# An mLSTM-and-two-MLPs kernel: every weight's low part moves to GpSimd, the weight rounding on ScalarE moves up within its step, and two tiles' attention pieces move one step later

## The reference, cut to what matters

```python
for t in range(S):
    m_new = np.maximum(f_gate[:, :, t] + m, i_gate[:, :, t])
    f_stab = np.exp(f_gate[:, :, t] + m - m_new); i_stab = np.exp(i_gate[:, :, t] - m_new)
    C = f_stab * C + i_stab * outer(v_t, k_t);  n = f_stab * n + i_stab * k_t
    y[:, :, t] = sigmoid(o_gate_t) * (C @ q_t) / max(|n @ q_t|, 1)
xn = x / rms(x) * rms_g                       # x: 1536 tokens of 320
x  = (silu(xn @ w_gate) * (xn @ w_val)) @ w_out     # 1536 hidden units
h  = x @ w_in
out = np.maximum(0.01 * h, h) @ w_out2              # 2048 hidden units
```

## Time and profile before

| | |
|---|---|
| time, three runs | 450.92, 450.02, 449.75 us; median 450.02 us |
| profiled execution: its own time, its span | 449.68 us, 447.9 us |
| mean granted clock of PE over the span | 0.996 |
| PE busy | 427.0 us, 95% of the span |
| PEld / DVE / ACT / POOL busy | 374.9 / 235.0 / 195.1 / 90.9 us |
| chain that ended last | PE 83%; ACT 5%; issue 4%; DVE 3%; POOL 3%; DMA 2% |

### The profile page before, as it was taken

The page is one execution under the profiler, slowest core; times in us unless marked ns, Lnnn a source line. Parts: engine busy times, 40 slices in busy tenths (PEclk is TensorE's granted clock), DMA queues, the critical chain, the costliest instruction groups (busy, mean ns, idle before and its releaser), DMA issues.

```text
span 447.9 us, 8151 instructions
## 1 busy us (share of the span) xinstructions
PE 427.0 (95%) x3202; PEld 374.9 (84%) x3202; DVE 235.0 (52%) x442; ACT 195.1 (44%) x428; POOL 90.9 (20%) x92
## 2 busy tenths in 40 slices
PE   2869989999999999999999999999999999999997
PEld 1758889999878878887888888998999999999996
DVE  7676666566649555555633335354334333543534
ACT  1758485455536435234333225554343343333332
POOL 1459685122111112000433102540000000000000
PEclk9989999999999999999999999999999999999999
DMA  5867581133303050000222200310000000010101
GB/s 169 299 235 236 156 304 51 75 123 122 122 1 121 1 173 1 1 0 0 66 64 69 61 0 15 118 32 0 1 0 1 0 2 0 10 50 1 59 1 59
DMA packets 10756, 31.37 MB, mean 70 GB/s; under 512 B 1328, under 2 KB 3088, under 8 KB 10720
## 3 DMA queue, kind: packets, MB, share of 16 engines
q1 hardware_dynamic: 10720, 30.87, 21.2%
HBM read 28.85 MB, written 2.02 MB: 69 GB/s over the span
## 4 chain that ended last, share of the span: by engine, by line
PE 83%; ACT 5%; issue 4%; DVE 3%; POOL 3%; DMA 2%; POOLq 0%; DVEq 0%; ACTq 0%
PE gate_ps L1033 23%; PE value_ps L1033 23%; PE out_ps L1070 9%; PE out_ps L1106 9%; PE turn_ps L1106 6%; PE out_ps L1074 3%; PE c_ps L1106 3%; PE turn_ps L1008 2%; ACT expo L486 2%; PE turn_ps L969 2%; POOL w_sb L423 1%; PE turn_ps L986 1%; ACT w_sb L539 1%; DMA expo<-decay_scratch 1%; PE c_ps L998 1%
## 5 line engine op out<-in xcount | busy, mean ns | idle before, releaser
L1033 PE MATMUL gate_ps<-x_hi,w_sb 128*128 128x512 f32 (+1 forms) x280 | 68.5, 366 | 3.8 <-DVE act_buf L811 1.9
L1033 PE MATMUL value_ps<-x_hi,w_sb 128*128 128x512 f32 (+1 forms) x280 | 68.4, 366 | 0.0
L1033 PEld LDWEIGHTS gate_ps<-x_hi,w_sb 128*128 128x128 f32 x280 | 46.9, 188 | 12.7 <-issue 3.3
L1033 PEld LDWEIGHTS value_ps<-x_hi,w_sb 128*128 128x128 f32 x280 | 47.6, 190 | 6.7 <-DVE hid L817 0.2
L559 ACT ACTIVATE h_hi<-hid 128x512 fp32r<-128x512 f32 (+1 forms) x46 | 24.6, 535 | 63.6 <-DVE hid L817 63.4
L811 DVE SCALAR_TENSOR_TENSOR act_buf<-act_buf,gate_ps 128x512 f32<-128x512 f32 (+1 forms) x46 | 26.1, 567 | 49.6 <-ACT act_buf L545 49.6
L836 DVE TENSOR_TENSOR h_lo<-hid,h_hi 128x512 fp32r<-128x512 f32 x48 | 33.2, 692 | 33.7 <-ACT h_hi L564 33.7
L1070 PE MATMUL out_ps<-h_hi,w_sb 128*128 128x512 f32 (+1 forms) x184 | 48.1, 347 | 0.0
L564 ACT ACTIVATE h_hi<-hid 128x512 fp32r<-128x512 f32 x48 | 30.3, 632 | 37.6 <-DVE hid L824 36.5
L545 ACT ACTIVATE act_buf<-gate_ps 128x512 f32<-128x512 f32 (+1 forms) x46 | 23.0, 500 | 48.6 <-PE gate_ps L1033 48.4
L1106 PE MATMUL out_ps<-w_sb,h_hi 128*128 128x320 f32 x192 | 43.0, 309 | 0.2 <-DVE h_lo L836 0.2
(11 more groups left out here) (142 smaller groups left out, 787.0 us busy)
## 6 DMA issues: line engine op xcount, KB each, us to landing
raw<-in_w SPq DMA_DIRECT2D x12, 544.0 KB, 4.4
expo<-decay_scratch SPq DMA_DIRECT2D x12, 512.0 KB, 5.3
att_sb<-in_tok SPq DMA_DIRECT2D x12, 484.0 KB, 5.0
raw<-in_w SPq DMA_DIRECT2D x16, 352.0 KB, 3.0
att_sb<-in_qk SPq DMA_DIRECT2D x24, 160.0 KB
out_y<-y_acc SPq DMA_DIRECT2D x12, 160.0 KB, 1.9
consts_sb<-in_consts SPq DMA_DIRECT2D x1, 129.5 KB, 2.5
gates_sb<-in_gates SPq DMA_DIRECT2D x1, 96.0 KB, 2.5
```

Source lines behind the costliest of these rows:

```text
L1033: last = nc.tensor.matmul(ps[:, 0:n], lhs, rhs, start=(j == 0), stop=(j == len(xs) - 1))
```

## The change

Five edits. (1) `lo_first` on DVE is gone; POOL makes block 1's low part behind the second `inverse_rms`, and `wait_lo` counts with one semaphore. (2) On POOL, `lo_weights(6)` and `inverse_rms(2)` stand ahead of `weigh_keys(3)`. (3) On ACT, `hi_weights(s + 3)` stands right behind the tangent `first1(s)` and no longer at the end of step s, and `high1(0)` stands behind `hi_weights(3)` and tile 2's first decays. (4) In `BESIDE`, tile 3's S moves from 3 to 4, tile 4's R from 8 to 9 and its O from 9 to 10 (so that its `normalise` is now `at_once`). (5) On DVE, `finish(n)` stands ahead of the second half of `scores` where both fall into one step.

```diff
@@ -32,7 +32,7 @@
 LAST1 = [max(s for s, (t0, _, _) in enumerate(STEPS) if t0 < (c + 1) * CHUNK_TILES) for c in range(CHUNKS)]
 
 
-BESIDE = {2: (1, 2, 3, 4), 3: (3, 5, 6, 7), 4: (7, 8, 9, 11), 5: (10, 12, 13, 14), 6: (14, 15, 16, 17),
+BESIDE = {2: (1, 2, 3, 4), 3: (4, 5, 6, 7), 4: (7, 9, 10, 11), 5: (10, 12, 13, 14), 6: (14, 15, 16, 17),
           7: (17, 18, 19, 20), 8: (20, 21, 22, 23), 9: (23, 24, 25, 26), 10: (26, 27, 28, 29),
           11: (29, 30, 31, 32)}
 
@@ -68,7 +68,6 @@
 GROUPS = 2
 GF = NF2 // GROUPS
 
-DVE_W = 1
 EARLY_W = 4
 
 EXPO = 3
@@ -210,7 +209,7 @@
         tab_done = sem("tab_done")
         exp_tab = sem("exp_tab")
         w_hi = sem("w_hi")
-        w_lo_dve = sem("w_lo_dve")
+
         w_lo = sem("w_lo")
 
         arg_done = sem("arg_done")
@@ -264,9 +263,7 @@
 
         def wait_lo(eng, i):
 
-            if i >= DVE_W:
-                eng.wait_ge(w_lo_dve, 1)
-            eng.wait_ge(w_lo, i + 1 if i < DVE_W else i)
+            eng.wait_ge(w_lo, i + 1)
 
         def cols1(s):
             t0, tiles, _ = STEPS[s]
@@ -437,6 +434,7 @@
             lo_weights(0)
             inverse_rms(0)
             inverse_rms(1)
+            lo_weights(1)
             exponents(2)
             lo_weights(2)
             lo_weights(3)
@@ -445,9 +443,9 @@
             lo_weights(4)
             fade_state(2)
             lo_weights(5)
+            lo_weights(6)
+            inverse_rms(2)
             weigh_keys(3)
-            inverse_rms(2)
-            lo_weights(6)
             lo_weights(7)
             exponents(4)
             lo_weights(8)
@@ -601,10 +599,10 @@
             x_high(1)
             hi_weights(2)
             first1(0, width(0))
-            high1(0)
             hi_weights(3)
             for n in beside(1)["S"]:
                 decay(n, 0)
+            high1(0)
             for s in range(1, STEPS1 + 1):
                 work = beside(s - 1)
                 if LAST1[-2] < s - 1 <= LAST1[-2] + GF:
@@ -613,6 +611,8 @@
                     first1(s, width(s))
                 else:
                     first2(s, s % RING)
+                if EARLY_W + s - 1 < NF1:
+                    hi_weights(EARLY_W + s - 1)
                 for n in beside(s - 2)["O"] if s >= 2 else ():
                     if not at_once(n):
                         normalise(n)
@@ -631,8 +631,6 @@
                     decay(n, 0)
                 for n in work["R"]:
                     ogate(n)
-                if EARLY_W + s - 1 < NF1:
-                    hi_weights(EARLY_W + s - 1)
                 if s - 1 in LAST1:
                     x2_high(LAST1.index(s - 1))
 
@@ -690,14 +688,6 @@
             dve.wait_ge(tab_ps, 2)
             nc.vector.tensor_copy(a_tab[:, :], out_ps[1][:, 0:TILES * H]).then_inc(tab_done, 1)
             nc.vector.tensor_copy(c_tab[:, NG:], out_ps[1][:, TILES * H + NG:2 * TILES * H]).then_inc(tab_done, 1)
-
-            def lo_first(i):
-                dve.wait_ge(w_hi, i + 1)
-                w, r = w1_sb[:, i, :], raw[:, i % RAW, :]
-                nc.vector.tensor_tensor(w[:, LO1:LO1 + W1M], r[:, 0:W1M], w[:, 0:W1M].bitcast(F32),
-                                        ALU.subtract)
-                nc.vector.tensor_tensor(w[:, LO_ODD:LO_ODD + ODD], r[:, W1M:W1RAW],
-                                        w[:, W1M:W1RAW].bitcast(F32), ALU.subtract).then_inc(w_lo_dve, 1)
 
             def bcast(tab, n, width):
                 return tab[:, n * H:(n + 1) * H].unsqueeze(2).broadcast_to([P, H, width])
@@ -884,7 +874,6 @@
             x_low(0)
             x_low(1)
 
-            lo_first(DVE_W)
 
             gated(0, width(0))
             hidden1(0, width(0))
@@ -897,10 +886,10 @@
                     denominator(n)
                 if s < STEPS1:
                     gated(s, width(s))
+                for n in work["O"]:
+                    finish(n)
                 for n in work["S"]:
                     scores(n, 1)
-                for n in work["O"]:
-                    finish(n)
                 for n in work["R"]:
                     from_state(n)
                 if s < STEPS1:
```

## The result

| | before | after |
|---|---|---|
| time, median (range), us | 450.78 (449.74 to 451.38, 10 runs) | 448.67 (446.74 to 449.72, 10 runs) |
| profiled execution, us | 449.68 | 448.65 |
| span, us | 447.9 | 446.9 |
| ratio of the times | | 0.9959, 95% interval 0.9947 to 0.997 |

A forecast was written before the change was run, and what follows sets the result against it. PE bounds the kernel, busy 427.0 of 447.9 us, with 5.1 us of waits addressed. Cumulative gains of 1.65 at gate(2), 2.6 after gate(6) and 3.5 at tile 5's scores gave 449.68 - 3.45 = 446.2, taken as 446.3; range 444.5 to 448.8.

The forecast's parts named there:

- the wait of R of tile 3 for `x_low`: Steps 6 to 11: rounding 8 ahead of `x_high` makes R wait 0.5 us, cutting the gain from 3.1 to 2.6.
- The step that failed: DVE's h_lo beside POOL's low parts: a blocked one ends 0.28 us behind POOL's instruction; a free one takes 0.43.
- the lock of h_lo(6): Steps 6 to 11: h_lo(6) meets POOL, but PE has R, an out product and scores between; not late.
- the forecast 70.5: Tile 5's scores on PE start at 70.5 instead of 73.98, a gain of 3.5 us.
- the 3.45: Whole kernel: the gain in us subtracted from the profiled execution of 449.68.
- The second term: Clock in the opening: full from 30.34, gate(1) loses 0.35 us; gain 0.9, or 0.5 if a microsecond later.
- B: Rival: only the opening pays, roundings ahead of `x_high` and blocked h_lo eat the rest; 1.65 left, 448.0 us; chance 0.16.
- the opening: Start of the kernel through step 1: gate(2) at 33.05 against 34.69, a gain of 1.65 us.
- C: Rival: all 5.1 us of PE waits go, as clock and `x_low` come earlier; 444.6 us; chance 0.12.
- D: Rival: slower, in the narrow steps each h_lo finds a POOL subtraction just begun; six of nine give 453.2 us; chance 0.06.
- E: Rival: nothing gained, a load of `raw` comes late to the earlier rounding and ACT stands; 449.7 us; chance 0.06.

The follow-up runs named there:

- e1: Changed kernel, with POOL waiting for h_lo(3) before block 6's low part; 447.21 us, ratio 0.9931.
- e3: Changed kernel, with the rounding behind `x_high` instead of ahead of it in the two steps with transposes; 448.49 us, ratio 0.9964.
- e4: Changed kernel plus ten small PE products, results unused, ahead of the second transposes and gate(0); 448.50 us, ratio 0.9946.
- e2: Changed kernel, with POOL waiting for h_lo(0), h_lo(3) and h_lo(6) ahead of blocks 3, 6 and 9; 446.74 us, ratio 0.9914.
- e5: Changed kernel, POOL waiting for h_lo(0), (3), (6), (8) ahead of blocks 3, 6, 9 and tile 5's mask, `x_high` ahead of the rounding; 445.89 us, ratio 0.9895.
- e7: e5 plus five small PE products, results unused, to keep the clock full; 445.78 us, ratio 0.9903.
- e10: e7 with block 4's load ahead of the load of tile 3's decays; 445.16 us, ratio 0.9891.
- u3: Changed kernel with only edit 3 undone: roundings at step ends, `high1(0)` directly behind the first tangent; 449.28 us, ratio 0.9971.
- e9: Changed kernel with POOL subtracting the 64 columns ahead of the 1024 in every weight block; 449.25 us, ratio 0.9981.
- e6: Changed kernel with a one-column memset on POOL between the low parts of blocks 5 and 6, no waiting; 448.01 us, ratio 0.994.
- e8: Changed kernel, POOL waiting for h_lo(0), (3), (6), (8) ahead of blocks 3, 6, 9 and tile 5's mask, rounding still ahead of `x_high`; 446.30 us, ratio 0.9911.

## Why the prediction was half right

Right, with the measured value: gate(1) 29.75 (29.64 predicted), no DVE row between 26.96 and 28.70, h_lo(0) 1.60 us (1.5), the wait of R of tile 3 for `x_low` 0.63 us (0.5), POOL's block 6 more than 4 us ahead of its gate. In the changed kernel's profile no rounding waits for its DMA, as predicted, but it is a near thing: with block 1 on POOL too, some rounding waits 0.48 us in e1, 0.63 in e3 and 1.58 in e4.

**The step that failed** is the one by which a blocked h_lo "ends 0.28 us behind POOL's instruction". It was read from one case, in which DVE got the first handover. Before's trace has three more blocked h_lo (at 35.85, 38.96 and 43.12, of 0.74, 1.22 and 0.79 us), and all end 0.28 us behind POOL's instruction: up to 80 us it holds none that was passed over, so it could not have shown the failure. The prediction applied it to h_lo(0), (5), (6) and (8) and charged h_lo(3) nothing. By the rule h_lo(3) would have ended at 42.43. It ended at 45.10, because block 6, moved forward by the change itself, stood directly behind block 5. Of these 2.67 us, 1.28 reach gate(6), and the lock of h_lo(6), which the prediction let PE cover with R and the scores, costs 0.57 at tile 3's transposes (e2 against after, with the same gate(2)). That is 1.85 of the 2.2 us by which tile 5's scores miss the forecast 70.5, and the 2.2 are most of what the profile misses of the 3.45 (it has 1.03). The ratios agree: 0.9914 for e2, 0.9959 for the change.

The second term was the clock, the rest of that sum. It came full at about 31.9 instead of 30.34, so gate(1) ran wholly and value(1) in part at 1.2 GHz, and gate(2) was 0.74 us later than predicted; some 0.5 of it is the clock's to give back (e4, e3), and 0.36 was left of that from gate(6) on. I had bounded it with a rise one microsecond late; it was 1.6. Nothing shows that it is the change's: the programs of e1, e5 and the kernel after are the same up to there but for one wait on POOL in e5, and the clock rose at 29.8 in e1's execution, at 31.9 here and not yet at 32 in e5's. The Trainium skill ("TensorE: Matmul & The Clock Gate", "Part 1: The HAM clock gate") calls the moment run-variable. These traces agree. The moment of one execution, 30.34, was no number to carry over.

The third is small: from gate(12) to the end the kernel after takes 370.05 us, before 369.85. Value(12) follows its gate after 1.08 us instead of 0.96, behind hidden1(11), and tile 4's transposes lose another 0.1. And one slip of arithmetic: 449.68 - 3.45 is 446.2, and with the 0.3 that the median was to lie above it 446.5, not 446.3.

The rivals. B ("only the opening pays") came nearest in its number, 448.0, for another reason: in the profiles the opening paid 0.90 of its 1.65, and 0.35 came behind it. That the time lies within the range is luck in the same way, since its upper end was set by B. C fell. D had the mechanism, DVE behind whole POOL subtractions, and priced six of 2.25 us; two that mattered came (1.28 and 0.57 at PE), not enough to make it slower. I set against D that an h_lo meets POOL at a random point. That is not so: the change fixes which POOL instruction stands beside which h_lo, and the order of both queues shows it. E happens in full when edit 1 is undone (u1, slower by 0.22%), and in part in most of the other versions (0.48 us in e1, 1.14 in e7, 1.83 in e10).

By the rule of the Trainium skill ("SBUF — State Buffer", "SBUF: two separate sides") the loser blocks fully for a whole instruction. The traces agree for the 1024-column pieces, but 3.07 and 3.37 us are longer than any one POOL instruction beside them, so the block can last over several. The mask, which reads and writes SBUF as well, locks too: the h_lo at 52.25 took 1.03 us beside the mask of 51.91 to 53.01.

How the edits share the gain, by ratio: edit 1 alone 0.9966, with edit 3 0.9991, with edits 2, 4 and 5 0.9971, all 0.9959, all but edit 1 1.0022. They don't add. Edit 1 alone reaches nearly all of the ratio, though 0.34 us only between the profiles. Edit 3 is worth 0.12% by the ratios, with intervals that overlap; whether it is worth more once POOL is held back for DVE was not tried.

**Open.** Why DVE gets the port at one handover (h_lo(0), h_lo(2), and in e1 and u3 h_lo(3)) and is passed over at another, two or three times in a row, I could not settle: neither nearness (e9) nor a memset between (e6) decides it. In e1 and u3 block 6 could not follow at once; but at 53.01 in the kernel after DVE got the port with 1024 columns ready behind the mask (they took 2.55 us, not 2.40). A fourth buffer for `raw`, which might take the loads out of e10, was not tried.

## What to carry to other kernels

When an edit fills one engine's queue, look at which instruction of it will stand beside each short one of an engine that shares its port, and count the one behind it too, not only the current one. Where the long instruction has slack, a one-line wait that holds it back until the short one is through costs next to nothing; four of them gave here some 2.2 us more than the change did (e8, by the ratios), from a place that no busy share shows. An earlier operand is worth something only if its buffer and its load come earlier as well.

## What the hardware showed that I had not expected

- The block of a port can outlast the instruction that caused it: 3.07 us (after), 3.00 (e6), 3.37 (e9), where POOL's single instructions beside them take 0.09 to 2.41.
- Locks may be what makes the time scatter: the runs of the kernel after span 3.0 us, those of e2 1.3, of e8 0.6, of e5 0.15. But e7, with the same holds as e5, spans 2.9, and in the kernel before the scatter goes with the mean granted clock (449.74 us at 0.996, 450.93 at 0.987 to 0.989), which is a rival, so this is a guess.
- A one-column power on POOL does not block: after's h_lo at 48.30 took 0.43 us beside the one of 48.04 to 48.59, as in the earlier trace rows.
- The recorded clock can be wrong. In e8 it reads 1.00 from 25 us on, but the durations are those of half speed: gate(0) to gate(1) 3.69 us, four matmuls in 1.05 or 1.19 us, where at the full clock 2.73 (e4) and 0.64 or 0.71 were seen. e9 has the same: 1.00 recorded, 3.69 us from gate(0) to gate(1). Windows, then PE of e8:

```profile
28.00:29.00 1.00, 1.00 (x6) 1.00 (x6) 0.13 (x1) 0.54 (x2) 1.00 (x1) 1.00 1.04 340
```

```profile
26.24 1.19 PE L1026 MATMUL gate_ps<-x_hi,w_sb 128*128 128x256 f32 x4 [1.01 <-issue]
...
29.93 1.05 PE L1026 MATMUL gate_ps<-x_hi,w_sb 128*128 128x256 f32 x4
```

The start-to-start time of equal products is the safer reading of the clock.
